# A scan kernel whose keys are scaled by feature and whose pairs of products are joined in 128 contraction rows

## What is computed

```python
def _attn_ref(r, k, v, w, a, b):                  # 4 x 8 heads, S = 768, D = 40
    state = np.zeros((B, H, D, D))
    for t in range(S):
        y[:, :, t] = np.einsum('bhd,bhde->bhe', rt, state)
        Sa = np.einsum('bhde,bhe->bhd', state, at)
        state_decay = state * wt[:, :, None, :] - np.einsum('bhd,bhe->bhde', Sa, bt)
        state = state_decay + np.einsum('bhd,bhe->bhde', vt, kt)

x = y.transpose(0, 2, 1, 3).reshape(B, S, 320)
h = x.transpose(0, 2, 1) @ U @ V                  # mixing over time, rank 32
u = x + h.transpose(0, 2, 1)
x2 = u + np.maximum(u @ w_ch1, 0.0) @ w_ch2       # 320 -> 1280 -> 320
# then causal attention of 4 experts (64 wide) on x2, each scaled by a top-2 gate
```

## Time and profile before

| | |
|---|---|
| median of three runs | 1131.28 us (1129.7 to 1132.03) |
| the profiled execution | 1122.77 us, span 1121.0 us |
| TensorE busy | 1031.1 us (92%), 23,184 matmul records |
| TensorE weight loads | 761.6 us (68%) |
| VectorE busy | 578.9 us (52%) |
| ScalarE busy | 431.4 us (38%) |
| GpSimd busy | 334.9 us (30%) |

### The profile page before, as it was taken

How to read it: one execution, slowest core, us unless ns; L and a number is a source line. 1 busy time by engine, 2 the same in 40 slices (tenths; PEclk the granted TensorE clock), 3 DMA queues, 4 the chain that set the end, 5 groups by cost and what they waited for, 6 DMA issues and landing times. The chain is left out here.

```text
span 1121.0 us, 51494 instructions
## 1 busy us (share of the span) xinstructions
PE 1031.1 (92%) x23184; PEld 761.6 (68%) x23184; DVE 578.9 (52%) x1272; ACT 431.4 (38%) x1207; POOL 334.9 (30%) x564
## 2 busy tenths in 40 slices
PE   4888877999998999999999899899999899999987
PEld 4777766666766787666766687666666787655556
DVE  5877864343344886144435787433334777110275
ACT  3766652322122555322222456422122455310155
POOL 4545555323232443023332444213232430000000
PEclk9999998999999999999999999999999999999989
DMA  7133233223212222112111223102110111000000
GB/s 235 58 93 116 89 110 86 81 72 111 56 55 60 68 78 70 40 41 54 60 59 47 68 71 93 58 25 67 41 47 23 49 42 55 22 0 1 1 12 25
DMA packets 47993, 68.37 MB, mean 61 GB/s; under 512 B 19744, under 2 KB 34848, under 8 KB 47776
## 3 DMA queue, kind: packets, MB, share of 16 engines
q1 hardware_dynamic: 47776, 65.09, 19.3%
HBM read 57.19 MB, written 7.86 MB: 58 GB/s over the span
## 5 line engine op out<-in xcount | busy, mean ns | idle before, releaser
L561 POOL TENSOR_TENSOR QI<-R,consts 128x256 f32<-128x256 f32 x180 | 144.8, 813 | 452.9 <-DVE R L780 422.1
L780 DVE COPY R<-PB 128x512 f32<-128x512 f32 (+1 forms) x147 | 95.4, 654 | 102.7 <-PE PB L1051 96.1
L656 ACT COPY R<-PB 128x512 f32<-128x512 f32 (+1 forms) x111 | 64.7, 583 | 201.2 <-PE PB L1051 197.7
L1332 PE MATMUL PB<-uf,W 128*128 128x384 f32 x320 | 111.7, 496 | 0.6 <-issue 0.6
L1364 PE MATMUL PB<-work,W 128*128 128x384 f32 x320 | 107.7, 490 | 1.1 <-issue 1.1
L1043 PEld LDWEIGHTS PB<-R 64*64 64x64 f32 x4032 | 72.3, 138 | 38.5 <-issue 26.7
L1043 PE MATMUL PB<-R 64*64 64x64 f32 x4032 | 86.7, 226 | 9.9 <-DVE UP L839 3.8
L968 DVE TENSOR_SCALAR work<-PB 128x384 f32<-128x384 f32 x40 | 22.3, 558 | 134.3 <-PE PB L1339 82.3
L1332 PEld LDWEIGHTS PB<-uf,W 128*128 128x128 f32 x320 | 58.2, 190 | 46.4 <-issue 12.1
L1364 PEld LDWEIGHTS PB<-work,W 128*128 128x128 f32 x320 | 59.4, 190 | 39.8 <-issue 1.4
L747 ACT COPY work<-PB 128x512 f32<-128x512 f32 (+3 forms) x128 | 53.2, 444 | 51.6 <-PE PB L1429 51.0
(11 more groups left out here) (154 smaller groups left out, 2112.0 us busy)
## 6 DMA issues: line engine op xcount, KB each, us to landing
EA<-ea_dram SPq DMA_DIRECT2D x48, 498.0 KB, 3.5
LA<-la_dram SPq DMA_DIRECT2D x48, 384.0 KB, 3.5
VT<-vt_dram SPq DMA_DIRECT2D x48, 80.0 KB, 2.6
x_mid_dram<-XO SPq DMA_DIRECT2D x192, 20.0 KB, 1.9
xs<-x_mid_dram SPq DMA_DIRECT2D x24, 160.0 KB, 3.2
out_dram<-work SPq DMA_DIRECT2D x24, 160.0 KB, 1.8
W<-w_dram SPq DMA_DIRECT2D x7, 320.0 KB, 5.0
W<-w_dram SPq DMA_DIRECT2D x1, 1280.0 KB, 8.5
```

The lines of the kernel that those rows point to most:

```text
L561: nc.gpsimd.tensor_tensor(QI[j][:].rearrange("p (u g t) -> p u g t", u=2, g=2), src.rearrange("p u (g t) -> p u g t", g=2), eye3.unsqueeze ...
L656: freed(nc.scalar.copy(tile[:, 8 * C:8 * C + hi], ps[:, 1, 0:hi]), group, i)
L780: freed(nc.vector.tensor_copy(tile[:, lo:hi], PB[PLACE[group, i][0]][:, 0, lo:hi]), group, i)
L1332: mm = nc.tensor.matmul(b_[:, j, 0:HW], W1[:, f, lo:lo + P], uf[:, f, j * HW:(j + 1) * HW], start=(f == 0 and m % 2 == 0), stop=(f == 1 an ...
```

## The change

1. Keys by feature. The products b and k over P are made in the layout with features in partitions: INV is now the reciprocal of the scan's own result shifted by one step, and of END for the last column, 128x252 and 128x4; GpSimd multiplies with b and k by feature (128x256 twice) to `BKf`. The step den, its tile and PT's third part go. The turned form `BK` is made from `BKf` by the same four transposes and one copy, which is now needed later only (for ST and o3, and no longer for s3).
2. 128 contraction rows. In `BK` the rows are b of the 64 steps over k of the 64 steps. X (upper half, copied by ACT) and V (lower half, by a new DMA `xv`, 128 KB a chunk) stand in `XV`. The state update (L1210) and the output product (L1241) are then eight matmuls each and not sixteen, in 128x64 tiles. The attention product (L1228) has X and V of a head side by side as 128 stationary columns (`xvf`, in LA): eight matmuls of 64x128 tiles and not sixteen of 64x64.
3. X comes out of its solve (L1200) in the upper half only, in two banks, and is turned by four transposes of 64 rows (L1219) and not two of 128.
4. Mixing: x is turned by transposes of its own ("xt", L1335), copied by ACT, and the product z V (u, L1342) is added by DVE.
5. The orders `FIRST_PERIOD`, `LAST_PERIOD` and `PERIOD` change; END is made on GpSimd at the place of the scan. `Pf` has three buffers, `BKf` two.

```diff
-LEAD = {"scan": 3, "bk": 2, "den": 2, "inv": 2,
+LEAD = {"scan": 3, "bk": 2, "inv": 2,
...
-PERIOD = ("A1", "A2", "mix", "A3", "B1", "scan", "den", "B3", "B2", "mix", "C1", "C2", "C3", "inv", "bk", "mix")
...
-FIRST_PERIOD = ("A3", "B3", "scan", "B4", "den", "A1", "B1", "C2", "T42", "B2", "inv", "bk", "A2", "C1", "C4", "C3", "T31")
...
+PERIOD = ("A1", "A2", "mix", "A3", "B1", "scan", "B3", "B2", "mix", "C1", "C2", "C3", "inv", "bk", "mix")
...
+FIRST_PERIOD = ("inv", "B4", "A1", "B1", "bk", "A3", "C2", "T42", "B3", "scan", "B2", "A2", "C1", "C4", "T31", "C3")
...
             def invert(n):
-                dve.wait_ge(den_made, n + 1)
                 if n >= 1:
                     dve.wait_ge(bk_made, 2 * n)
-                nc.vector.reciprocal(INV[:], DEN[:]).then_inc(inv_made, 1)
+                nc.vector.reciprocal(gt(INV[:])[:, :, 0:C - 1], gt(at(Pf, n)[:])[:, :, 1:C]).then_inc(inv_made, 1)
+                dve.wait_ge(ended, n + 1)
+                nc.vector.reciprocal(gt(INV[:])[:, :, C - 1:C], at(END, n)[:].unsqueeze(2)).then_inc(inv_made, 1)
...
+            def make_bk(n):
+                pool.wait_ge(inv_made, 2 * n + 2)
+                if n >= BKF_DEPTH:
+                    taken(pool, "s3", n - BKF_DEPTH)
+                    taken(pool, "s2", n - BKF_DEPTH)
+                out = at(BKf, n)[:].rearrange("p (x j t) -> p x j t", x=4, j=2)
+                for j in range(2):
+                    nc.gpsimd.tensor_tensor(out[:, :, j], gt(bk(n, j)), gt(INV[:]), ALU.mult).then_inc(bk_made, 1)
...
             def update(n, out):
+                pe.wait_ge(xv_in[n % XV_DEPTH], 16 * (n // XV_DEPTH) + 16)
+                taken(pe, "s2", n)
                 taken(pe, "X", n)
                 for g, p, u in HEADS:
-                    col = 6 * C + g * D
-                    mm = nc.tensor.matmul(out[feat(u), p, col:col + D], at(BK, n)[half(p), spaced(g, u)],
-                                          XS[half(p), spaced(g, u)], start=False, stop=True, skip_group_check=True)
+                    lo, key, col = head(g, p, u), key_of(g, p, u), 6 * C + g * D
+                    mm = nc.tensor.matmul(out[feat(u), p, col:col + D], at(BK, n)[:, key:key + D],
+                                          at(XV, n)[:, lo:lo + D], start=True, stop=True)
                 return mm
...
             def features(n, out):
...
-                for g in range(2):
-                    mm = nc.tensor.transpose(out[:, 0, g * P:(g + 1) * P], XS[:, g * P:(g + 1) * P], ident)
+                for x in range(4):
+                    mm = nc.tensor.transpose(out[:, 0, x * C:(x + 1) * C], at(XV, n)[half(0), x * P:(x + 1) * P],
+                                             ident[half(0), half(0)])
...
             def attention(n, out):
                 pe.wait_ge(la_in[n % 2], 16 * (n // 2) + 16)
                 taken(pe, "o1", n)
-                for x in range(2):
-                    for g, p, u in HEADS:
-                        t_ = (2 * p + g) * C
-                        left = (XF[feat(u), g * P + p * C:g * P + p * C + C], vfu(n)[feat(u), t_:t_ + C])[x]
-                        lo = (2 * x + g) * C
-                        mm = nc.tensor.matmul(out[half(p), u, lo:lo + C], left, rfu(n)[feat(u), t_:t_ + C],
-                                              start=True, stop=True)
+                for g, p, u in HEADS:
+                    x = 2 * p + g
+                    mm = nc.tensor.matmul(out[:, u, x * C:(x + 1) * C], xvf(n)[feat(u), x * P:(x + 1) * P],
+                                          rfu(n)[feat(u), x * C:(x + 1) * C], start=True, stop=True)
...
-                for j in range(2):
-                    for g, p, u in HEADS:
-                        lo, key, col = u * 4 * C + (2 * j + g) * C, j * 4 * C + (2 * g + u) * C, TOK + g * D
-                        mm = nc.tensor.matmul(out[half(p ^ u), u, col:col + D], WS[half(p), lo:lo + C],
-                                              at(BK, n)[half(p), key:key + D], start=False, stop=(j == 1),
-                                              skip_group_check=True)
+                for g in range(2):
+                    for p, u in ((0, 0), (0, 1), (1, 1), (1, 0)):
+                        lo, key, col = (4 * u + 2 * p + g) * C, key_of(g, p, u), TOK + g * D
+                        mm = nc.tensor.matmul(out[half(p ^ u), u, col:col + D], WS[:, lo:lo + C],
+                                              at(BK, n)[:, key:key + D], start=False, stop=True, skip_group_check=True)
...
                 elif what == "u":
...
-                    for i in range(HW // P):
-                        nc.tensor.matmul(b_[:, i * P:(i + 1) * P], xs[:, j * (HW // P) + i, f * P:(f + 1) * P],
-                                         ident, start=(i == 0), stop=False, skip_group_check=True)
-                    mm = nc.tensor.matmul(b_[:, 0:HW], z[:, f * P:(f + 1) * P], Vw[:, j * HW:(j + 1) * HW],
-                                          start=False, stop=True, skip_group_check=True)
+                    is_out(pe, "z", n)
+                    mm = nc.tensor.matmul(b_[:, 0:HW], z[:, f * P:(f + 1) * P], Vw[:, j * HW:(j + 1) * HW], start=True,
+                                          stop=True)
```

More of the change, by code:

```diff
@@ L129, in mixing_steps @@
 def mixing_steps(b):
-    mixing = ([("z", b), ("u", b, 2)] + [("u", b, f, n) for n in range(NH) for f in range(2)]
+    blocks = [(f, n) for n in range(NH) for f in range(2)]
+    mixing = ([("xt", b, *blocks[0]), ("xt", b, *blocks[1]), ("z", b), ("xt", b, *blocks[2]), ("xt", b, *blocks[3]),
+               ("u", b, 2)] + [("u", b, f, n) for f, n in blocks]
               + [("h", b, m) for m in range(NM)]
@@ L358, in program @@
         vt_in = [sem(f"vt_in{j}") for j in range(VT_DEPTH)]
+        xv_in = [sem(f"xv_in{j}") for j in range(XV_DEPTH)]
         consts_in, x_in = sem("consts_in"), sem("x_in")
@@ L506, in _ @@
                             load_la(m)
+                        for m in range(XV_DEPTH):
+                            load_xv(m)
                 elif what == "h" and i == 0 and args[0] % 2 == 0:
@@ L551, in _ @@
         def _(pool):
-            for rows in (XS, ST[0], ST[1], *BK):
+            for rows in ST:
                 nc.gpsimd.memset(rows[:], 0.0).then_inc(padded, 1)
+            for rows in XV:
+                nc.gpsimd.memset(rows[half(0), :], 0.0).then_inc(padded, 1)
             pool.wait_ge(consts_in, 16)
-            pool.wait_ge(padded, 3 + BK_DEPTH)
+            pool.wait_ge(padded, PADDED)
             eye3 = eye.unsqueeze(1)
@@ L628, in _ @@
                         make_qi(5, late, R25, 4 * C)
-                elif what == "den":
-                    make_den(i + LEAD["den"])
+                elif what == "scan":
+                    make_end(i + LEAD["scan"])
                 elif what == "C1":
@@ L972, in _ @@
                         freed(nc.vector.tensor_tensor(ur[:], b_[:, 0:HW], ur[:], ALU.add), *step)
-                    elif what == "x2":
+                    elif what in ("u", "x2") and args[0] < 2:
                         is_full(dve, *step)
                         f, j = args
+                        if what == "u":
+                            is_out(dve, "xt", n, f, j)
                         sl = slice(j * HW, (j + 1) * HW)
@@ L1157, in removed @@
                 else:
[L1158 removed]
+                    pe.wait_ge(padded, PADDED)
                 for g, p, u in HEADS:
@@ L1308, in _ @@
                     filled(mm, *step)
+                elif what == "xt":
+                    b_ = turn(*step)
+                    f, j = args
+                    pe.wait_ge(x_in, 16 * (NT * n + (HW // P) * (j + 1)))
+                    for i in range(HW // P):
+                        mm = nc.tensor.transpose(b_[:, i * P:(i + 1) * P], xs[:, j * (HW // P) + i, f * P:(f + 1) * P],
+                                                 ident)
+                    filled(mm, *step)
                 elif what == "u":
@@ L1463, in chunks, with by_feature, by_chunk @@
     return x.reshape(B, 2, 2, 2, NC, C, D)
-def by_feature(x, rows):
+def by_feature(x, rows, fill=0.0):
     y = chunks(x).transpose({"g": (0, 4, 2, 6, 3, 1, 5), "u": (0, 4, 2, 6, 1, 3, 5), "p": (0, 4, 1, 6, 2, 3, 5)}[rows])
-    return np.pad(y, ((0, 0),) * 3 + ((0, C - D),) + ((0, 0),) * 3)
+    return np.pad(y, ((0, 0),) * 3 + ((0, C - D),) + ((0, 0),) * 3, constant_values=fill)
+def by_chunk(x):
+    return chunks(x).transpose(0, 4, 5, 1, 3, 2, 6)
 def by_token(x):
```

140 lines of the change are left out of this document (72 added, 68 removed).

## The result

The changed kernel took 1162.57 us (median of four, 1154.48 to 1168.55) against 1131.57 us (1129.7 to 1132.03): a ratio of 1.029, 95% interval 1.024 to 1.034. That is 31.0 us slower, where 31 was forecast (1162.0, range 1138 to 1180). The profiled execution took 1156.6 us with a span of 1154.8; +33.8 us on the span of before. The four times are two pairs, 1154.48 and 1156.6 us with a granted clock of 0.975 and 0.973, and twice 1168.55 with 0.959 and 0.962; the median lies between them.

A forecast was written before the change was run, and what follows sets the result against it. Beside the mixing TensorE's own time was taken to bound the kernel, in the recurrence alone the turn of its loop; +29 and +2 us on the profiled 1122.77 gave 1153.8, as median 1162 us, range 1138 to 1180.

The forecast's parts named there:

- attention, 128 stationary columns: Attention product beside the mixing: eight pairs at 110 ns for eight packs at 58, +0.41 us a chunk, +15 us.
- 156 changes of tile shape: TensorE beside the mixing: 485 changes of tile shape become 641, at 137 ns each, +21 us.
- output product and update in 128 rows: Output product and state update: pairs cost the same 58 and 37 ns as the packs before, so zero.
- x turned by transposes: Mixing: 12 blocks a batch go from two records at 110 ns to one, -5 us.
- waits: +1 for the keys, -3 filled: Beside the mixing: +1 us where attention makes VectorE busy, -3 us for TensorE waits that added work fills.
- The turned X: X's two transposes of 109 ns become four at 53 to 110 ns: 0 to +0.2 us a chunk, taken as 0.
- The recurrence alone: Stretch without mixing: +0.4 us a period, +5 us, and -3 us at the start; sum +2 us, bounds -16 to +14.
- Attention at its stream: Rival: an attention pair costs 58 ns though its weights are 128 wide, so 15 us go: 1147; chance 0.14.
- The number of records decides: Rival: TensorE's time goes with its records, 14.6 ns for each dropped one, so faster, 1095 us; chance 0.06.
- The loop alone: Rival: the recurrence's period alone falls under 10.6 us, so faster or about the same, 1129 us or below; chance 0.08.
- The pairs do overlap: Denies a rival: 128x64 pairs don't overlap, output product and update rise up to 1.7 us a chunk, 1180 and more; chance 0.10.
- One sign that the prediction called wrong: Beside the mixing: VectorE's reciprocal as what TensorE or GpSimd waits for would show the prediction wrong; no size given.

The follow-up runs named there:

- xt_alone: The kernel before with only the mixing's transposes of x added; 1123.77 us, ratio 0.999 to the kernel before.
- keys_xt: The kernel before with transposes of x, keys by feature and the changed orders, all products as before; 1129.44 us, ratio 1.007.
- att64: The changed kernel with the attention product back in sixteen matmuls in 64x64 tiles; 1147.74 us, ratio 1.024 to the kernel before.
- b3_covered: xt_alone with the recurrence's full-tile transposes moved behind two other steps and ahead of a mixing step; 1127.9 us, ratio 1.003.
- b3_head: xt_alone with the recurrence's full-tile transposes moved to the head of the period; 1203.51 us, ratio 1.068.
- two_mixes: xt_alone with the full-tile transposes behind three other steps and the mixing in two places a period, not three; 1147.82 us, ratio 1.020.
- mix_in_two: b3_head with the mixing in two places a period, not three; 1195.78 us, ratio 1.061.
- n128: The changed kernel with 128 moving columns, not 64, in six of the attention product's eight matmuls; 1157.57 us in one run.
- recip_short: keys_xt with the first reciprocal at 160 columns, not 252; 1131.97 us in one run, beside 1127.86 for the kernel before.

## Why the prediction was right

By its own steps, beside the mixing (the first five rows are work, from the table):

| step | predicted | measured |
|---|---|---|
| attention, 128 stationary columns | +15 | +15 (pairs at 111 ns against packs at 58) |
| 156 changes of tile shape | +21 at 137 ns | +15 to +19, at 95 to 119 ns |
| output product and update in 128 rows | 0 | pairs 58 and 38 ns, as the packs |
| x turned by transposes | -5, with 1.3 behind the stretch | -4.0, and -1.8 behind it |
| keys by feature, TensorE's work | 0 | +1.0, within the noise |
| waits: +1 for the keys, -3 filled | -2 | idle -6.1, clock +4.7: -1.4 |

TensorE's work grew by 28.5 us where the sum had 32.3 (15 + 21 - 3.7): at 105 ns, 156 changes are 16 us and not 21. More idle time was filled than the sum had (6.1 us, not 3), and the clock, for which it had no term, took 4.7 us of that back. So the total (+27.1, where the prediction without the last stretch's share has +30) is near partly since misses cancel.

The experiments split the same 27.1 us by part: the transposes -2.9 (before to xt_alone), keys by feature with the new orders +6.1 (to keys_xt), update, output product and turned X in their new tiles +7.6 (to att64), attention's 128 columns +16.3 (to the changed kernel). The sum's +1 for the keys is thus far off where they stand alone. In the changed kernel, whose TensorE has 31.6 us more to do, idle time is 10.7 us shorter than in keys_xt; how much of the keys' price is left there was not measured.

That the median came out at 1162.57 where 1162.0 was forecast is luck in the last digits: it lies between two pairs of runs 12 to 14 us apart, and the profiled execution grew by 33.8 us, not 31.

The mis-sized term beside the mixing is the change of shape. I took 94 ns and 33 to 53 for a first load or stream. 94 was read behind full tiles; over all the changes made here the sum is nearer to 105, though around attention it is 145. Why it differs stays open.

*The turned X.* Its four transposes of 64 rows start 112, 63 and 61 ns after each other: behind the first about 60 ns each, near the stream that I took, not the 110 of the upper bound.

*The recurrence alone.* Predicted +0.4 us a period and -3 at the start. Measured 11.7 and not 11.5 us a period, and -2.5: the first products start at 10.3 us, the prediction had 10.1 for 12.97. What it had no term for is the end of that stretch, +9.1 us, where the granted clock is 0.84 (0.91 before) and TensorE's idle time 13.4 us (9.5 before). Of the 9.1 us, 3.9 are idle time, 3.9 clock and 1.3 work. Its share in the sum is not fixed by this one profile. Six kernels keep the old order up to the mixing, and the stretch beside it begins in them at 197.0 (before), 203.1, 200.9, 205.1, 206.0 and 209.0 us (xt_alone, b3_covered, b3_head, two_mixes, mix_in_two). The changed kernel and its three variants with the same products have 205.6, 207.8, 206.2 and 210.9. The +8.6 us of the one pair is thus no larger than what kernels with one and the same order differ by; the means are 4 us apart. TensorE's work up to the mixing does tell them apart, 145.2 to 148.1 us against 137.5 to 143.9, which is rough here, since nearly a quarter of the stretch is idle; 64 changes at 105 ns and 12 x 0.41 would be 11.6. Which of the waits belong to the change stays open.

Two of the prediction's bounds don't follow from its own terms. With X turned at 110 ns (+0.2 us a chunk) the sum beside the mixing is some +36, not +42; and with all of the added 13.7 us on the loop alone and the start's -3, that stretch is +11, not +14.

*The rivals.* Attention at its stream fell with n128. The number of records decides: 1,686 fewer records beside the mixing came with 28.5 us more work. The loop alone did not shrink below 10.6 us. The pairs do overlap: 58 ns with 64 stationary columns. One sign that the prediction called wrong did show in the changed kernel: GpSimd waits for VectorE's reciprocal (INV), 12.3 us over the whole execution, 8.9 of them in eight waits beside the mixing. The first line is from the page of the profile, the second is the longest entry among TensorE's waits beside the mixing (total, times, longest):

```profile
L600 POOL TENSOR_TENSOR BKf<-EA,INV 128x256 f32<-128x256 f32 x96 | 69.9, 750 | 15.9 <-DVE INV L821 12.3
...
PE PB L1185 <- DVE R L802: 4.8, 6, 1.4
```

GpSimd is busy 226 of 786 us there, and TensorE waits neither for INV nor for BKf beside the mixing. Its own longest entry, 4.8 us, is for VectorE's copies of R. So the wait was there, and too small to turn the result.

The two rules that the prediction weighed: the load by stationary columns ("TensorE: Matmul & The Clock Gate", LDWEIGHTS, of the Trainium skill) agrees with the trace, 111 ns for 128 columns where an estimate by its formula is 107. The floor of 25 ns between matmuls of few columns that the same page of the Trainium skill states under "Back-to-back issue gap" doesn't hold with four tiles at once: 16 records of L1206 in 0.23 us, 14 ns each.

## What to carry to other kernels

Count packs (the matmuls that run at once, one in each tile), not instructions. With TensorE in tiles, a pack costs the larger of the stationary and the moving columns of one tile (40 and 40: 38 ns, 64 and 64: 58, 64 and 128: 109 in L1060, 128 and 64: 111, 128 and 128: 112), and filling more contraction rows at the price of half the tiles brings nothing; making weights 128 columns wide where only 64 columns stream doubles the price. Each change of tile shape costs about 0.1 us on top in the mean, so a shape of its own for a group of eight small products must save more than two changes.

And split a gain or a loss into work, waits and clock before explaining it. Here -4.5 us of work came with +6.3 us of length (b3_covered), and 3.9 us less idle time with 1.1 us less length (recip_short).

## What I had not expected of the hardware

The clock looks like part of the price of a wait. Beside the mixing, each fall to 1.2 GHz had 1.0 to 4.5 us of idle time of TensorE in the 7 us ahead of it, and cost 1.7 us or more in these kernels, about as much as the wait itself. The waits need not be long: ahead of the fall at 652.0 us in the changed kernel there were 1.7 us of them, the longest 0.8. The kernel with 82 us idle lost 34 us in this way (28 if idle time within the falls isn't counted), that with 30 us idle 6.8, though not in strict proportion: two_mixes has 56 us idle and lost 10.2. What separates a wait that costs the clock from one that doesn't was not tried.

In a 40x128 tile's pair with 128 stationary columns twice the moving columns change nothing (1.04 and 1.03 us for 16 records).
